# Attention on one core: the first group's inverse from 16x16 blocks, and paced first loads

## The chip, the core and the metric

One Trainium2 chip, and of it one core. Its engines run side by side, each through its own queue in order: TensorE (matrix products, PE in the profile, its weight loads PEld), VectorE (DVE), ScalarE (ACT), GpSimd (POOL) and SyncE (SP), which here issues the DMA transfers. They wait for each other by semaphores. The measure is the device time of one execution in microseconds; three runs stand at 898.11, 903.13 and 903.36, so the median is 903.13.

## The reference, cut to what matters

Attention with a delta rule runs ahead of two feed-forward stages, which the change doesn't touch. Batch 4, 8 heads, 768 tokens, head size 48:

```
k_n = k / (norm(k) + 1e-06)
for t in range(S):
    y[t] = q[t] @ state
    v_old = k_n[t] @ state
    state = state + beta[t] * outer(k_n[t], v[t] - v_old)
```

Its output, the heads side by side, goes into a spectral mixer with a feed-forward part (`mixer`) and then into a gated feed-forward part (`gated`).

## The kernel before, in words

`attention` works in chunks of C = 64 tokens. A chunk of one head is solved in closed form: with G the products of its normalised keys (a gram matrix), the recurrence inside it is a unit lower triangular system, whose inverse T is needed before anything of the chunk can be computed. Two heads stand on the 128 partitions, U = 32 units (pairs of head and chunk) make a group, and there are six groups. A 64x64 inverse is made of four quarters of 32 rows: two diagonal 32x32 blocks, and a corner that comes from them by two products on TensorE.

Ahead of the main loop, and for later groups within it:

- `piece("g", g, p)` (line 423) multiplies a quarter of a group's keys with themselves, the gram; `piece("a", g, p)` keys with queries, the score. Each is 16 matmuls of 64x64, into one of two PSUM banks that take turns by the list `uses`. ScalarE drains each (lines 314 and 318).
- `to_lanes` (558) transposes the diagonal blocks, gathered in `g_diag`, so that each of 32 units times 4 quarters has a lane of its own. Group 0's blocks are copied out of `gram_sb` by VectorE (618), ScalarE (353) and GpSimd (282), later groups' by DMA (`diagonal`, 185).
- `lanes` finds the norms (ScalarE gives the root, 307) and scales; `column` (599, 603) then solves the 32x32 blocks by forward substitution, 31 columns of two operations each, every one waiting for the one before it through the semaphore `chain`. In column 24 (`AHEAD`), `to_lanes` of the next group is done. `unlanes` (610, 612) transposes back into `t_rows` and `t_cols`.
- `couple_w` (435) and `couple_x` (448) form the corner on TensorE, in halves of 16 units; ScalarE puts the parts into `tt` (325, 336, 346).

The main loop has 48 steps, 8 for each group, on TensorE and ScalarE: u (492), y (509, 514), s (527) and r (474) of four units a step, each drained by ScalarE. VectorE meanwhile does the inverse of group g + 1. Blocks and couplings of later groups stand between the steps: at group 0's steps only `g` blocks of group 3 and, at the last step, `couple_w(1, 0)`. SyncE's list of loads is written by hand, each held back by a `wait_ge` on what frees its buffer or on a place in `chain`. GpSimd masks the scores (`causal`, 246), scales v (`scaled`, 253) and clears `t_lane` (`clear`, 260).

## Time and profile before

| | |
|---|---|
| median of three runs | 903.13 us (898.11 to 903.36) |
| profiled execution, its own time | 899.3 us |
| its span | 897.5 us |
| mean granted TensorE clock | 0.928 |
| attention, first to last step | up to about 260 us |
| group 0's inverse on VectorE | 13.2 to 49.1 us |
| group 0's steps on TensorE | 58.4 to 79.7 us |

The span is that of the instructions; the execution's own time has what lies around it as well. In the profile an instruction has a start and a duration in microseconds, and the engine's idle time ahead of it with what ended it. A granted clock of 1.00 is TensorE's 2.4 GHz, 0.50 its 1.2 GHz. A 32-bit matmul shows as two records, so 16 matmuls are 32 records.

### The profile page before, as it was taken

The numbers are of one execution on the slowest core, as the hardware profiler recorded it, in microseconds if no ns is written. First come the engines' busy times: TensorE is split into PE (matmuls) and PEld (weight loads), VectorE is DVE, ScalarE is ACT, GpSimd is POOL, SyncE is SP. The second block draws the span as 40 slices with busy tenths as digits, with TensorE's granted clock in tenths as the row PEclk, the third lists the DMA queues.
The fourth block names the chain that finished last, engine by engine and source line by source line (L and its number), as shares of the span: only waits on it lengthen the run. The fifth ranks groups of instructions, "written<-read, shape, count | busy, mean of one in ns | idle before, by whom it ended". The sixth has DMA issues, their size and how long they took to land.

```text
span 897.5 us, 24703 instructions
## 1 busy us (share of the span) xinstructions
PE 834.6 (93%) x10634; PEld 809.9 (90%) x10634; DVE 475.1 (53%) x1092; ACT 301.3 (34%) x654; POOL 199.4 (22%) x167
## 2 busy tenths in 40 slices
PE   7368999999984999999999999999999999999998
PEld 6368989899884999999999999999899899899898
DVE  5999999999295554435443443333632432432421
ACT  4246575675431221122111211123441431431421
POOL 3123123023001803600540000000132222222231
PEclk9758779697886999999999999999999999999999
DMA  6633454422564030012000103003410010000001
GB/s 198 163 121 99 148 148 119 132 58 74 158 215 131 3 123 19 18 54 70 18 18 14 56 18 116 20 15 105 152 53 27 27 53 27 26 0 27 27 1 53
DMA packets 38074, 65.14 MB, mean 73 GB/s; under 512 B 4249, under 2 KB 26082, under 8 KB 37986
## 3 DMA queue, kind: packets, MB, share of 16 engines
q1 hardware_dynamic: 37986, 63.85, 22.7%
q8 instruction: 69, 1.13, 0.5%
q14 instruction: 19, 0.16, 0.1%
HBM read 46.86 MB, written 14.16 MB: 68 GB/s over the span
## 4 chain that ended last, share of the span: by engine, by line
PE 61%; issue 20%; DVE 11%; ACT 4%; POOL 2%; DMA 1%; SPq 1%; POOLq 0%; ACTq 0%; DVEq 0%
PE m_ps_h L1111 13%; PE g_ps_v L1622 11%; PE m_ps_d L1111 11%; PE ps_ga L423 4%; PE g_ps_y L1622 3%; PE g_ps_u L1622 3%; PE ps_y L509 3%; PE ps_y L514 2%; PE ps_u L492 2%; DVE t_lane L603 2%; DVE prod L599 2%; PE ps_r L474 2%; ACT tt L346 2%; PE ps_s L527 2%; POOL g_vn_lo L1519 2%
## 5 line engine op out<-in xcount | busy, mean ns | idle before, releaser
L1111 PE MATMUL m_ps_h<-m_unt_hi,m_w_hi 128*128 128x256 f32 x432 | 122.7, 284 | 2.1 <-DVE m_unt_lo L1301 2.1
L1111 PE MATMUL m_ps_h<-m_unt_lo,m_w_hi 128*128 128x256 f32 x432 | 121.9, 282 | 0.0
L1111 PE MATMUL m_ps_h<-m_unt_hi,m_w_lo 128*128 128x256 f32 x432 | 121.8, 282 | 0.0
L1307 DVE SCALAR_TENSOR_TENSOR m_h_lo<-m_ps_h,m_h_hi 128x512 fp32r<-128x512 f32 x72 | 49.8, 692 | 107.8 <-ACT m_h_hi L1011 107.8
L1111 PE MATMUL m_ps_d<-m_w_hi,m_h_hi 128*128 128x384 f32 x288 | 97.6, 339 | 0.0
L1111 PE MATMUL m_ps_d<-m_w_hi,m_h_lo 128*128 128x384 f32 x288 | 96.4, 335 | 0.0
L1111 PE MATMUL m_ps_d<-m_w_lo,m_h_hi 128*128 128x384 f32 x288 | 96.3, 334 | 0.0
L1011 ACT ACTIVATE m_h_hi<-m_ps_h 128x512 fp32r<-128x512 f32 x72 | 43.1, 598 | 151.0 <-PE m_ps_h L1111 151.0
L1111 PEld LDWEIGHTS m_ps_h<-m_unt_hi,m_w_hi 128*128 128x128 f32 x432 | 82.4, 191 | 2.6 <-DVE m_unt_lo L1301 2.5
L1111 PEld LDWEIGHTS m_ps_h<-m_unt_hi,m_w_lo 128*128 128x128 f32 x432 | 83.5, 193 | 0.0
L1111 PEld LDWEIGHTS m_ps_h<-m_unt_lo,m_w_hi 128*128 128x128 f32 x432 | 82.5, 191 | 0.0
L603 DVE TENSOR_TENSOR t_lane<-t_lane,prod 128x31 f32<-128x31 f32 (+15 forms) x186 | 66.3, 356 | 6.4
L423 PE MATMUL ps_ga<-kq 64*64 64x64 f32 x1536 | 59.4, 235 | 10.6 <-DMA kq<-kq_g 8.3
L599 DVE TENSOR_TENSOR prod<-g_lane,t_lane 128x31 f32<-128x31 f32 (+15 forms) x186 | 63.7, 343 | 6.2
L1783 DVE TENSOR_TENSOR g_vs<-g_ps_v,g_bias 128x384 f32<-128x384 f32 x32 | 17.9, 558 | 92.3 <-PE g_ps_v L1622 92.0
L1519 POOL TENSOR_TENSOR g_vn_lo<-g_vn,g_vn_hi 128x512 fp32r<-128x512 f32 x24 | 30.5, 1286 | 161.5 <-ACT g_vn_hi L1561 161.5
L423 PEld LDWEIGHTS ps_ga<-kq 64*64 64x64 f32 x1536 | 56.2, 150 | 11.2 <-DMA kq<-kq_g 4.4
L1622 PE MATMUL g_ps_v<-g_ws_hi,g_vn_hi 128*128 128x384 f32 x192 | 64.4, 335 | 0.0
L1622 PE MATMUL g_ps_v<-g_ws_hi,g_vn_lo 128*128 128x384 f32 x192 | 64.1, 334 | 0.0
L1622 PE MATMUL g_ps_v<-g_ws_lo,g_vn_hi 128*128 128x384 f32 x192 | 64.1, 334 | 0.0
L1525 POOL TENSOR_TENSOR g_g<-g_vs,g_ut 128x384 f32<-128x384 f32 x32 | 36.7, 1147 | 114.0 <-DVE g_vs L1783 114.0
L514 PE MATMUL ps_y<-u_sb,score 64*64 64x48 f32 x768 | 60.9, 246 | 0.0
(220 smaller groups left out, 1963.5 us busy)
## 6 DMA issues: line engine op xcount, KB each, us to landing
kq<-kq_g SPq DMA_DIRECT2D x48, 256.0 KB, 3.6
v_in<-v_g SPq DMA_DIRECT2D x12, 384.0 KB, 4.2
k_in<-k_g SPq DMA_DIRECT2D x12, 384.0 KB, 3.6
x_scr<-y_sb SPq DMA_DIRECT2D x24, 192.0 KB, 2.9
stage<-w_ch SPq DMA_DIRECT2D x6, 768.0 KB, 4.8
x_scr<-m_x_sb SPq DMA_DIRECT2D x24, 192.0 KB, 1.9
g_x<-x_scr SPq DMA_DIRECT2D x24, 192.0 KB, 4.5
out<-g_y SPq DMA_DIRECT2D x24, 192.0 KB, 1.9
```

The lines of the kernel that those rows point to most:

```text
L346: last = act.activation(tt[g % 2][quarter(a), :, H * (a % 2):H * (a % 2) + H], t_cols[quarter(a)], ACT.Copy)
L423: last = pe.matmul(ps_ga[m % 2][lo:lo + C, C * j:C * j + C], x[:, 0], x[:, 0 if what == "g" else 1], start=True, stop=True)
L509: pe.matmul(ps_y[out, at:at + D], kq[g % 4][lo:lo + C, 1, PR * m + j], s_sb[lo:lo + C, b, j], start=True, stop=False)
L514: last = pe.matmul(ps_y[out, at:at + D], score[g % 2][rows, PR * m + j], u_sb[rows, j0 % 2, j], start=j0 < NB, stop=True)
L599: dve.tensor_tensor(x, g_lane[g % 2][:, j + 1:H, j].unsqueeze(2).broadcast_to([P, m, n]), t_lane[:, j, 0:n].unsqueeze(1).broadcast_to([P, ...
L603: dve.tensor_tensor(below, below, x, ALU.add).then_inc(chain, 1)
L1011: act.activation(h_hi[:, 2 * g:2 * g + 2], ps_h[g % 2][:, :].rearrange("p (f t) -> p f t", f=2), ACT.Relu).then_inc(h_hi_ok, 1)
L1111: last = pe.matmul(out, first[x], second[y], start=(k == 0 and m == 0), stop=(k == n - 1 and m == 2))
L1307: dve.scalar_tensor_tensor(h_lo[:, 2 * g:2 * g + 2].rearrange("p f t -> p (f t)"), ps_h[g % 2][:, :], 0.0, h_hi[:, 2 * g:2 * g + 2].rearra ...
L1519: pool.tensor_tensor(vn_lo[:, t], vn[:, t % 2], vn_hi[:, t].bitcast(F32), ALU.subtract).then_inc(vn_lo_ok, 1)
L1525: pool.tensor_tensor(g[:, n % 2], vs[:, n % 2], ut[:, f, HS * h:HS * h + HS], ALU.mult).then_inc(g_ok, 1)
L1622: last = pe.matmul(out, first[x], second[w], start=(k == 0 and m == 0), stop=(k == n - 1 and m == 2))
```

## The change

Group 0 alone gets another inverse. Its four gram blocks have a PSUM bank each (`ps_four`, four banks that `ps_y` and the two turning banks lie in), and VectorE and ScalarE copy the diagonal blocks straight out of them, half by half, before ScalarE drains the grams. VectorE's lanes invert only the two 16x16 blocks on the diagonal of each 32x32 block (`fine_column`, 15 columns instead of 31, both blocks in one operation). With D their inverse and L the block below them, TensorE forms V = I - L D (`fine_v`) and then D V (`fine_inverse`), which is the 32x32 inverse, and its transpose for two quarters. ScalarE's `below` makes L out of `g_diag` by a factor of -1 or 0 for each partition.

Only the first half of group 0's units gets all that ahead of the loop. The second half's `fine_v`, `fine_inverse`, `couple_w` and `couple_x` stand at steps 1 to 4 of it. So do the four score blocks of group 1, at steps 2 to 5. The first loads go in pairs, each pair waiting for the landing of the pair two before it; the loads of group 1's queries come after them. `to_lanes(1)` follows `unlanes(0)`. The table that the square root needs is loaded at the start. The rest of the kernel is as it was.

```diff
-    FIRST = (("g", 0), ("a", 0), ("g", 1), ("a", 1), ("g", 2))
+    FIRST = (("g", 0), ("g", 1), ("a", 0), ("g", 2))
...
+        def links(g):
+            return FINE_LINKS + (g - 1) * LINKS if g else 0
...
+            sp.wait_ge(kq_in[0][0][0], 32)
+            for s, g in ((0, 1), (1, 0), (0, 2)):
+                for c in range(2):
+                    sp.wait_ge(kq_in[0 if (s, g) == (0, 1) else 1 if s else 0][0 if s or g == 1 else 1][c], 32)
+                    for p in (2 * c, 2 * c + 1):
+                        load_kq(g, s, p)
+            sp.wait_ge(kq_in[2][0][1], 32)
             diagonal(1)
...
+            for p in range(4):
+                sp.wait_ge(chain, links(1) + 2 + 6 * p)
+                load_kq(1, 1, p)
...
-                pool.wait_ge(chain, g * LINKS + 2 * AHEAD + 4)
+                pool.wait_ge(chain, links(g) + 2 * AHEAD + 4 if g else links(1))
...
+            act.wait_ge(one_ok, 1)
+            act.activation(one[:, 1:2], one[:, 0:1], ACT.Sqrt)
+            for c in range(2):
+                act.wait_ge(ga_done, 2 * c + 2)
+                for a in (1, 3):
+                    act.activation(g_diag[quarter(a), HU * c:HU * c + HU], first_gram(quarter(a), c, 1),
+                                   ACT.Copy).then_inc(dg_act, 1)
+            act.wait_ge(dg_dve, 4)
             for p in range(4):
                 piece("g", 0, p)
-            act.wait_ge(ga_out, 4)
-            act.activation(g_diag[quarter(1)], gram_sb[0][quarter(1), 1], ACT.Copy).then_inc(dg_act, 1)
+            roots(0)
...
+            def fine_v(c):
+                m = turn["v", 0, c]
+                bank_free(m)
+                pe.matmul(ps_ga[m % 2][:, 0:HU * H], ident[:], unit[:].unsqueeze(1).broadcast_to([P, HU, H]),
+                          start=True, stop=False, skip_group_check=True)
+                pe.wait_ge(below_ok, 1)
+                pe.wait_ge(trows_ok, 1)
+                for j in range(HU):
+                    for a in range(4):
+                        u = HU * c + j
+                        last = pe.matmul(coupling(m, quarter(a))[:, j], below[quarter(a), u], t_rows[quarter(a), u],
+                                         start=False, stop=True, skip_group_check=True)
+                last.then_inc(ga_done, 1)
+            def fine_inverse(c):
+                m = turn["c", 0, c]
+                bank_free(m)
+                pe.wait_ge(tcols_ok, 1)
+                pe.wait_ge(ga_out, turn["v", 0, c] + 1)
+                for j in range(HU):
+                    for a in range(4):
+                        u = HU * c + j
+                        last = pe.matmul(coupling(m, quarter(a))[:, j], v_fine[quarter(a), u], t_cols[quarter(a), u],
+                                         start=True, stop=True)
+                last.then_inc(ga_done, 1)
+                m = turn["r", 0, c]
+                bank_free(m)
+                for j in range(HU):
+                    for a in (0, 2):
+                        u = HU * c + j
+                        last = pe.matmul(coupling(m, quarter(a))[:, j], t_cols[quarter(a), u], v_fine[quarter(a), u],
+                                         start=True, stop=True)
+                last.then_inc(ga_done, 1)
...
+                if k == 1:
+                    fine_v(1)
+                if k == 2:
+                    fine_inverse(1)
+                if 2 <= n < 6 and i + 1 < G:
                     piece("a", i + 1, n - 2)
...
-                if i and n == 1:
+                if n == (1 if i else 3):
                     couple_w(i, 1)
-                if i and n == 2:
+                if n == (2 if i else 4):
                     couple_x(i, 1)
...
+            def fine_column(j):
+                m, n = Q - 1 - j, j + 1
+                x = prod[:, 0:2 * m * n].rearrange("p (b i k) -> p b i k", b=2, k=n)
+                g, t = diagonal_pair(g_lane[0]), diagonal_pair(t_lane)
+                rest = t[:, :, j + 1:Q, 0:n]
+                dve.tensor_tensor(x, g[:, :, j + 1:Q, j].unsqueeze(3).broadcast_to([P, 2, m, n]),
+                                  t[:, :, j, 0:n].unsqueeze(2).broadcast_to([P, 2, m, n]), ALU.mult).then_inc(chain, 1)
+                dve.wait_ge(chain, 2 * j + 3)
+                dve.tensor_tensor(rest, rest, x, ALU.add).then_inc(chain, 1)
+                dve.wait_ge(chain, 2 * j + 4)
```

TensorE from its first instruction to the loop's first three steps, before the change (`ps_ga<-kq` are the blocks, `ps_u`, `ps_y`, `ps_s` the steps):

```order
L423 MATMUL ps_ga<-kq 64x64 x320
L435 MATMUL ps_ga<-t_rows,gram_sb 32x32 x64
L448 MATMUL ps_ga<-t_cols,w_sb 32x32 x64
L492 MATMUL ps_u<-v_in,tt 64x48 x16
L514 MATMUL ps_y<-u_sb,score 64x48 x8
L527 MATMUL ps_s<-u_sb,k_in 48x48 x8
L492 MATMUL ps_u<-v_in,tt 64x48 x8
```

and with the change, as far as the second u (`w_sb` under line 546 is `below`, `score` under 559 and 567 is V):

```order
L500 MATMUL ps_four<-kq 64x64 x256
L539 MATMUL ps_four<-unit,ident 128x512
L546 MATMUL ps_four<-t_rows,w_sb 32x32 x64
L559 MATMUL ps_four<-t_cols,score 32x32 x64
L567 MATMUL ps_four<-score,t_cols 32x32 x32
L515 MATMUL ps_four<-t_rows,gram_sb 32x32 x32
L531 MATMUL ps_four<-t_cols,w_sb 32x32 x32
L612 MATMUL ps_u<-v_in,tt 64x48 x8
L539 MATMUL ps_four<-unit,ident 128x512
L546 MATMUL ps_four<-t_rows,w_sb 32x32 x64
L612 MATMUL ps_u<-v_in,tt 64x48 x8
```

Sixty-four of the score blocks' matmuls have left the start, half of the couplings too, and the first `fine` products stand ahead of the loop, the others between its first two u.

TensorE, steps 2 to 4 of group 0 before the change, from the second y:

```order
L514 MATMUL ps_y<-u_sb,score 64x48 x8
L527 MATMUL ps_s<-u_sb,k_in 48x48 x8
L466 MATMUL ps_r<-v_in,ident 128x192
L474 MATMUL ps_r<-s_sb,kq 64x48 x8
L492 MATMUL ps_u<-v_in,tt 64x48 x8
```

and with the change, from the first y:

```order
L634 MATMUL ps_four<-u_sb,score 64x48 x8
L647 MATMUL ps_s<-u_sb,k_in 48x48 x8
L559 MATMUL ps_four<-t_cols,score 32x32 x64
L567 MATMUL ps_four<-score,t_cols 32x32 x32
L500 MATMUL ps_four<-kq 64x64 x16
L612 MATMUL ps_u<-v_in,tt 64x48 x8
L634 MATMUL ps_four<-u_sb,score 64x48 x8
L647 MATMUL ps_s<-u_sb,k_in 48x48 x8
L500 MATMUL ps_four<-kq 64x64 x16
L515 MATMUL ps_four<-t_rows,gram_sb 32x32 x32
L586 MATMUL ps_r<-v_in,ident 128x192
L594 MATMUL ps_r<-s_sb,kq 64x48 x8
```

Between the steps stand now the other half of `fine_inverse`, two score blocks of group 1 and the coupling.

ScalarE at steps 3 and 4 of group 0 with the change (`u_sb`, `s_sb`, `y_sb`, `r_sb` are a step's drains, line 405 is `first_corners`, line 371 `solved_x`):

```order
L360 ACTIVATE w_sb<-ps_four 128x512 [waits ga_done]
L405 ACTIVATE tt<-t_cols 32x16x32 [waits tt_zero,ga_out]
L405 ACTIVATE tt<-t_cols 32x16x32 x3
L437 ACTIVATE r_sb<-ps_r 128x192 [waits p_done]
L441 ACTIVATE u_sb<-ps_u 128x192 [waits u_done]
L337 ACTIVATE ps_r<-v_in 128x192 [waits r_ok]
L453 ACTIVATE s_sb<-ps_s 128x192 [waits s_done]
L458 ACTIVATE y_sb<-ps_four 64x2x4x48 [waits y_done]
L353 ACTIVATE score<-ps_four 128x512 [waits ga_done]
L349 ACTIVATE gram_sb<-ps_four 128x8x2x32 [waits ga_done]
L371 ACTIVATE tt<-ps_four 32x16x32 [waits tt_zero,ga_done]
```

The four corner copies stand ahead of step 4's drains; before the change they, and every coupling drain of group 0, stood ahead of the loop.

## Rows read from the trace of the kernel before

**Rows 1.** The page's part 1: busy us, share of the span, instructions.
```profile
PE 834.6 (93%) x10634; PEld 809.9 (90%) x10634; DVE 475.1 (53%) x1092; ACT 301.3 (34%) x654; POOL 199.4 (22%) x167
```

**Rows 2.** Busy time by stretches: length; PE, PEld, DVE, ACT, POOL; clock, DMA share, GB/s.
```profile
45.20:58.30 13.10, 6.90 (x256) 6.79 (x256) 12.25 (x29) 7.64 (x10) 5.92 (x5) 0.50 0.19 62
58.30:70.10 11.80, 11.33 (x199) 10.56 (x201) 10.91 (x27) 4.08 (x12) 0.00 (x0) 0.50 0.57 175
70.10:79.60 9.50, 9.50 (x337) 9.42 (x333) 8.78 (x23) 6.56 (x19) 3.01 (x2) 1.00 0.45 134
...
81.20:101.50 20.30, 19.33 (x507) 18.76 (x509) 18.79 (x49) 12.06 (x24) 4.08 (x4) 0.58 0.46 136
...
120.00:160.30 40.30, 37.22 (x1155) 36.02 (x1154) 37.33 (x93) 25.37 (x59) 8.75 (x6) 0.83 0.44 128
```

**Rows 3.** Waits of TensorE, us in total, times, longest: 0 to 250, then 83.3 to 230.
```profile
PE ps_ga L435 <- DVE t_rows L610: 15.2, 2, 13.3
...
PE ps_u L492 <- ACT tt L346: 4.4, 4, 2.0
```

**Rows 4.** TensorE in order of time: start, duration, line, what, and its wait.
```profile
16.13 3.95 PE L423 MATMUL ps_ga<-kq 64*64 64x64 f32 x128 [0.74 <-ACT score L318]
...
28.64 5.50 PE L423 MATMUL ps_ga<-kq 64*64 64x64 f32 x128 [3.88 <-DMA kq<-kq_g]
47.42 3.47 PE L435 MATMUL ps_ga<-t_rows,gram_sb 32*32 32x32 f32 x122 [13.29 <-DVE t_rows L610]
...
58.35 1.09 PE L492 MATMUL ps_u<-v_in,tt 64*64 64x48 f32 x16 [4.03 <-ACT tt L346]
...
79.09 0.57 PE L423 MATMUL ps_ga<-kq 64*64 64x64 f32 x11
81.52 1.20 PE L435 MATMUL ps_ga<-t_rows,gram_sb 32*32 32x32 f32 x64 [1.86 <-DVE t_rows L610]
```

**Rows 5.** GpSimd and ScalarE in order of time, at group 2's inverse.
```profile
117.53 0.95 POOL L260 MEMSET t_lane<- 128x1024 f32 x1 [0.29 <-DVE t_cols L612]
...
122.02 2.11 ACT L346 ACTIVATE tt<-t_cols 32x1024 f32<-32x1024 f32 x2
```

**Rows 6.** VectorE in order of time, group 0's inverse.
```profile
10.99 2.13 DVE L618 COPY g_diag<-gram_sb 32x1024 f32<-32x1024 f32 x2 [8.98 <-ACT gram_sb L314]
...
15.63 0.35 DVE L568 RECIPROCAL rinv<-root 128x32 f32<-128x32 f32 x1 [0.30 <-ACT root L307]
...
17.72 1.22 DVE L589 SCALAR_TENSOR_TENSOR g_lane<-g_lane,scale 128x1024 f32<-128x1024 f32 x1
...
19.46 0.22 DVE L599 TENSOR_TENSOR prod<-g_lane,t_lane 128x60 f32<-128x60 f32 x1
19.71 0.22 DVE L603 TENSOR_TENSOR t_lane<-t_lane,prod 128x60 f32<-128x60 f32 x1
...
21.16 0.30 DVE L599 TENSOR_TENSOR prod<-g_lane,t_lane 128x135 f32<-128x135 f32 x1
21.50 0.30 DVE L603 TENSOR_TENSOR t_lane<-t_lane,prod 128x135 f32<-128x135 f32 x1
...
45.23 2.05 DVE L610 STREAM_TRANSPOSE t_rows<-t_lane 128x1024 f32<-128x1024 f32 x1
```

**Rows 7.** ScalarE in order of time: block drains, then corner drains.
```profile
30.19 0.60 ACT L314 ACTIVATE gram_sb<-ps_ga 128x512 f32<-128x512 f32 x1 [4.80 <-PE ps_ga L423]
31.90 0.60 ACT L314 ACTIVATE gram_sb<-ps_ga 128x512 f32<-128x512 f32 x1 [1.11 <-PE ps_ga L423]
...
53.71 2.40 ACT L336 ACTIVATE tt<-ps_ga 32x512 f32<-32x512 f32 x4
```

**Rows 8.** The page's part 6: DMA issues, KB each, us to landing.
```profile
kq<-kq_g SPq DMA_DIRECT2D x48, 256.0 KB, 3.6
```

**Rows 9.** GpSimd in order of time: the scaling of v for group 0.
```profile
38.98 2.77 POOL L253 TENSOR_TENSOR v_in<-v_in,norm 128x1536 f32<-128x1536 f32 x1 [26.40 <-DVE t_lane L603]
```

205 lines of the change are left out of this document (135 added, 70 removed).

## The prediction

> **What bounds the kernel now.** The page comes first. TensorE is busy 93% of the span and VectorE 53% [rows 1]. The edit touches only the first 120 us or so, and those shares say nothing of that stretch, so the next view is the table by stretches. In 58.3 to 70.1 and 70.1 to 79.6 TensorE is busy nearly throughout, first at a granted clock of 0.50 (1.2 GHz), then at 1.00 (2.4 GHz), while VectorE is busy over 90% as well [rows 2]. Busy shares can't tell which of the two sets the end. The list of waits can: TensorE waited for VectorE's `t_rows` twice, 13.3 us and 1.9 us (15.2 less 13.3), and from 83.3 to 230 us never again; there it waits for ScalarE's corner copies, 4.4 us over 4 waits [rows 3]. The 13.3 us end at 47.42, where group 0's inverse is ready, and the 1.86 us at 81.52, for group 1's [rows 4]. At group 2, VectorE's `t_cols` were done at 117.5 (GpSimd's clear of `t_lane` starts on them), and ScalarE came to its copies at 122.02 [rows 5]: VectorE is 4.5 us early. So VectorE bounds the program up to 81.5 us, and TensorE from there. **A VectorE that is 16 us earlier is worth only what TensorE can follow.** The quantity to forecast is when TensorE reaches the first matmul of `couple_w(1, 0)`, now 81.52. Everything behind it moves by the same amount.
>
> **VectorE, group 0.** It now waits for the last gram drain, then copies two 32x1024 quarters in 2.13 us, 10.99 to 13.12 [rows 6]; with 0.6 us for that drain the fourth block is done near 10.4. After: the first half is copied while the other is still being multiplied, and only two 32x512 copies from PSUM follow 10.4. ScalarE takes 2.40 us for four of that size [rows 7], 0.6 each, so 11.6, which is 1.5 us earlier. The square root then stands behind ScalarE's four gram drains (four in 2.2 us, 0.6 each less some overlap), so `rinv` starts at 14.1 where 15.63 stood: still 1.5. The two 16x16 scalings have 256 elements a lane each where 1024 took 1.22 us; a quarter of the elements twice saves 0.3 to 0.4. The columns: 62 operations with `to_lanes(1)` between them ran from 18.94 to 45.23. The new chain has 30 operations of 30 to 128 elements. Operations of 60 and 135 elements take 0.22 and 0.30 us, 0.25 and 0.34 from start to start [rows 6]; thirty at 0.245 to 0.325 make 8.6 us. So columns run 17.1 to 25.7, `t_rows` is ready at 27.8 (now 47.3), `t_cols` at 29.7. `to_lanes(1)`, 2.9 us, now follows instead of lying inside. Group 1's columns thus start some 16 us earlier. The 4-dimensional patterns of `fine_column` are in no row; were each operation 0.1 us slower, the chain would be 3 us longer, which then ties with the next item.
>
> **Loads.** In pairs that wait for each other, each about 3.6 us from issue to landing [rows 8], two pairs are under way at a time: landings near 4.4, 5, 8, 9, 11.5, 12.5, 15, 16. The uses (first blocks at 4.4, the second group's at 14, the last at 24) come later, so I take the pacing at nothing. What it could give is an earlier first block (a few tenths), what it could cost a late `diagonal(1)`, which sends four transfers and is queued behind the last pair and the drain of group 1's grams at about 20. Its data is needed at 29.7, so 7 us of cover. The v loads land near 27 and `scaled(0)` (2.77 us [rows 9]) lies beside the transposes; its `v_ok` is needed at 43. `load_kq(1, 1)` moved behind `chain` 34 (near 37), done landing by 45, needed at 48.
>
> **TensorE before the loop.** After the four gram blocks it stands until ScalarE has drained them (13.8). Then twelve blocks at 0.99 us (3.95 for four) plus 1.5 us for a start at 1.2 GHz, as after the gap before 28.64 [rows 4], then the 128x512 identity matmul, 1.35 us scaled from 192 columns: 28.6. So VectorE's result at 27.8 is no longer what it waits for. Now the join for half the units. Price: `couple_w(1, 0)`, 32 matmuls shown as 64 records, took 1.20 us at 2.4 GHz; 128 records took 3.47 at 1.2 GHz [rows 4], so 18.8 or 27 ns a record. `fine_v` (128 records) 2.4, copy 0.7, `fine_inverse` (192) 3.6 to 5.2, three copies 1.8 (0.6 each [rows 7]), `couple_w` 1.4, copy 0.6, four corner copies 2.4 covering `couple_x`, two more 1.2: 14.3 to 16, starting at 28.6. First u matmul at 43.5, where it was 58.35. Bounds: 41 if four corners at once run faster than two, 46 all at 1.2 GHz.
>
> **TensorE's loop over group 0.** It now takes 58.35 to 79.66, 528 records of 64-row matmuls. Moved in: four `a` blocks of group 1, 128 records; `fine_v(1)` and `fine_inverse(1)`, 320; `couple_w(0, 1)` and `couple_x(0, 1)`, 128; the second identity matmul. That is 656 of the one kind and 448 of the other. Rates: 337 records in 9.5 us at 2.4 GHz [rows 2], 35.5 a us; at 1.2 GHz one block of 32 per 1.71 us (the drains at 30.19 and 31.90 [rows 7]), 18.8 a us. At 2.4 GHz throughout: 18.5 + 8.4 + 1.4 + 0.5 (the 192-column identity matmul) = 28.8 us. At 1.2 GHz: 34.9 + 12.1 + 2.7 + 1.0 = 50.7 us. The trace has the loop at 1.2 GHz until 70.1, about 10 us behind its dense start at 60, and the next stretch, 81.2 to 101.5, averages 0.58, so 17 of its 20 us [rows 2]. I take 10 us: they do a fifth of the work, the rest takes 23.1, together 33.1. New waits, from ScalarE's order: the `a` block behind `fine_inverse(1)` waits for the `t_cols` copy (0.7); `couple_x(0, 1)` and the fifth u matmul wait behind the four corner copies that ScalarE does first, 1.3 and 0.6; 0.4 more for the rest. 3 us. So 43.5 + 33.1 + 3 = 79.6 against 81.5: **1.9 us gained.** Behind the next boundary, from 120 to 160.3, the clock averages 0.83: 13.7 us at 1.2 GHz, against 17 behind this one, which has the 1.86 us gap that now goes. I take 1 us for it (0 to 2). VectorE's group 1 is done at about 68 (its `unlanes` waits for `couple_x(0, 1)`, near 64), group 2 starts when ScalarE gives the root at step 6, near 70 where it was 83: 12 us early, not binding. The total is 3 us.
>
> The profiled run took 899.3, so 896.3 by its own sum. It lies 3.8 under the median of 903.13, and one of the three runs at 898.11; 903.1 - 3 = **900**.
>
> The Trainium skill ("TensorEngine Tiling (Array Packing)", Key Properties) says that 32x32 tiles execute independently and that a change of tiling mode drains TensorE. No row has four corners at once. By the first, 256 of the 320 fine records would shrink; by the second, the eight new switches between 64 and 32 rows in the loop would each cost something, against this change.
>
> **Rivals.**
> (1) Four corners overlap: if 256 records in each half take half as long, 2.4 us go from the start and 2.4 to 3.5 from the loop, and with the higher clock from 4 us on (as at 28.64) the loop takes 30.5: 40.9 + 30.5 - 3 + 3 = 71.4, a gain of 10 to 11 with the 1: 892. For it: four disjoint corners of the array. Against: two already alternate, and 18.8 ns may be the floor. 0.15. The page named above would have this.
> (2) Only the clock is better: high after 4 us, 43.5 + 30.5 + 3 = 77, gain 5.5: 897.5. 0.2.
> (3) VectorE's 16 us come through whole: 887. It would need TensorE's added work to be free; [rows 2] has no idle time for it. 0.04.
> (4) **Slower, by the clock in the loop.** The 32-row matmuls from 47.42 on ran at 0.50 to their end, 7 us of them [rows 2, 4]. In the loop they now stand at its beginning. If 1.2 GHz lasts t us, the loop ends at 43.5 + 3 + 28.8 + 0.43 t, which passes 81.5 at t = 14.4. With t = 25 it is 86, 4.6 later: 908 (0.17). With the whole loop at 1.2 GHz, 97.2, so 919 (0.05).
> (5) The early change doesn't do what it says: a paced load comes late at start, and VectorE's chain with it; up to 3 us at the start leaves about 0: 903. 0.04.
> The forecast has 0.35.
>
> **Numbers.** 1% is 9 us, about what a measurement can tell from no change. Faster by more: (3), most of (1), a little of (2), 0.21. Slower by more: (4)'s second case and a tail of its first, 0.08. Between: 0.71. The range takes in (1) with a little beyond and the first case of (4): 890 to 908.
>
> **What would show it.** The first u matmul near 43.5; `t_rows` at 28; `couple_w(1, 0)` near 79.6 with no wait for `t_rows` ahead of it; group 0's loop some 36 us long, of which 10 at 1.2 GHz; VectorE waiting for ScalarE's root, and idle more than before. Wrong if TensorE still waits for `t_rows` of group 1, if a fine record takes other than 18.8 to 27 ns, or if the stretch behind group 1 changes length by over 2 us.

## The result and the profile after

The changed kernel took 906.87 us (median of 20 runs, 900.66 to 910.82); the kernel before, on the same chip, 902.0 (20 runs, 897.22 to 907.13). The ratio is 1.0052, with a 95% interval of 1.003 to 1.0073: about 4.7 us slower, where 3 us of gain were forecast. The time lies inside the range, on the other side of no change. The profiled execution has a span of 905.3 against 897.5.

VectorE first, since the change is made for it: in order of time, start, duration, line, operation, then its wait.

```profile
12.10 1.93 DVE L681 STREAM_TRANSPOSE g_lane<-g_diag 128x1024 f32<-128x1024 f32 x1
...
16.65 0.75 DVE L717 SCALAR_TENSOR_TENSOR g_lane<-g_lane,scale 128x256 f32<-128x256 f32 x2
17.43 0.21 DVE L739 TENSOR_TENSOR prod<-g_lane,t_lane 128x30 f32<-128x30 f32 x1
...
21.80 0.29 DVE L742 TENSOR_TENSOR t_lane<-t_lane,prod 128x128 f32<-128x128 f32 x1
...
26.12 2.08 DVE L749 STREAM_TRANSPOSE t_rows<-t_lane 128x1024 f32<-128x1024 f32 x1
28.10 1.91 DVE L751 STREAM_TRANSPOSE t_cols<-t_lane 128x1024 f32<-128x1024 f32 x1
...
64.27 0.19 DVE L730 TENSOR_TENSOR t_lane<-t_lane,prod 128x31 f32<-128x31 f32 x1
74.78 2.05 DVE L749 STREAM_TRANSPOSE t_rows<-t_lane 128x1024 f32<-128x1024 f32 x1 [10.33 <-PE ps_four L531]
...
83.25 0.35 DVE L691 RECIPROCAL rinv<-root 128x32 f32<-128x32 f32 x1 [4.59 <-ACT root L342]
```

Beside [rows 6], `t_rows` of group 0 is ready at 28.2 in place of 47.3. The four-dimensional patterns of `fine_column` cost nothing extra (30 elements in 0.21 us, 128 in 0.29). VectorE ends group 1's columns at 64.46. It then waits 10.33 us for TensorE's `couple_x(0, 1)` and 4.59 us for ScalarE's root, and group 2 starts at 83.25, where it started before the change too. The whole lead is gone there, in waits for TensorE and for ScalarE behind it.

TensorE in order of time. The rows answer to [rows 4]; x is the number of records, and each f32 matmul shows as two.

```profile
28.47 0.95 PE L546 MATMUL ps_four<-t_rows,w_sb 32*32 32x32 f32 x89
31.40 0.54 PE L546 MATMUL ps_four<-t_rows,w_sb 32*32 32x32 f32 x39 [1.97 <-issue]
32.72 1.25 PE L559 MATMUL ps_four<-t_cols,score 32*32 32x32 f32 x89 [0.79 <-ACT score L388]
36.29 0.74 PE L559 MATMUL ps_four<-t_cols,score 32*32 32x32 f32 x37 [2.31 <-issue]
...
36.84 1.90 PE L567 MATMUL ps_four<-score,t_cols 32*32 32x32 f32 x63
40.59 1.92 PE L515 MATMUL ps_four<-t_rows,gram_sb 32*32 32x32 f32 x64 [1.84 <-ACT t_rows L396]
43.28 1.92 PE L531 MATMUL ps_four<-t_cols,w_sb 32*32 32x32 f32 x64 [0.78 <-ACT w_sb L360]
46.87 1.09 PE L612 MATMUL ps_u<-v_in,tt 64*64 64x48 f32 x16 [1.68 <-issue]
...
53.94 0.90 PE L559 MATMUL ps_four<-t_cols,score 32*32 32x32 f32 x83
57.70 0.80 PE L559 MATMUL ps_four<-t_cols,score 32*32 32x32 f32 x43 [2.86 <-issue]
...
76.01 0.57 PE L612 MATMUL ps_u<-r_sb,tt 64*64 64x48 f32 x13 [0.74 <-issue]
...
86.36 1.07 PE L515 MATMUL ps_four<-t_rows,gram_sb 32*32 32x32 f32 x56
```

The join starts when it was forecast to, at 28.47. Three times it stops in the middle of a run of equal matmuls, 1.97, 2.31 and 2.86 us long, with no releaser ("issue"). From 31.40 to 36.29 lie 39 + 89 = 128 records. (The 1.68 us ahead of the first u matmul are named "issue" as well, but are the wait for ScalarE's last two corner copies. So are the 0.74 us ahead of the fifth u matmul at 76.01: ScalarE's copies of the second half end at 75.92.)

```profile
74.73 1.19 ACT L371 ACTIVATE tt<-ps_four 32x512 f32<-32x512 f32 x2 [0.82 <-PE ps_four L531]
```

`couple_w(1, 0)`, whose first matmul the forecast was about, starts at 86.36. It stood at 81.52 in [rows 4], and 79.6 was forecast. Busy time by stretches, the join and then the loop over group 0: length; PE, PEld, DVE, ACT, POOL (instructions); clock, DMA share, GB/s.

```profile
28.40:46.80 18.40, 9.10 (x449) 8.37 (x448) 16.61 (x38) 6.53 (x12) 8.19 (x6) 0.62 0.28 87
46.80:86.40 39.60, 33.63 (x1110) 30.87 (x1112) 23.14 (x52) 19.26 (x46) 8.74 (x6) 0.79 0.40 122
```

The same loop before the change, with less in it:

```profile
58.30:81.50 23.20, 20.89 (x530) 19.99 (x531) 21.59 (x50) 11.24 (x32) 4.91 (x3) 0.74 0.50 153
```

TensorE is idle 9.3 us of the join's 18.4 and 6.0 us of the loop's 39.6. The page's part 3 (DMA queue, its kind: packets, MB, share) has 69 packets of instructions before:

```profile
q8 instruction: 69, 1.13, 0.5%
```

and 74 after:

```profile
q8 instruction: 74, 1.21, 0.6%
```

Part 1 has 11278 TensorE records in place of the 10634 in [rows 1]: 644 more, and five packets more. That is one packet of 16 KB for each 129 records, or 128 within what so small a count can tell. The theory taken into the experiments is **A**: TensorE's instructions come in such pieces, and a piece that is worked off faster than the next one comes leaves TensorE standing.

### The profile page after: what moved, and what is told of

Its sections match the earlier page's. It is cut to its first block, busy times and chain, and to the rows that moved or that the text cites. A ratio compares the mean times of both kernels' runs of the same rounds, so it can differ in the third digit from the quotient of the medians.

```text
span 905.3 us, 25993 instructions
## 1 busy us (share of the span) xinstructions
PE 840.6 (93%) x11278; PEld 812.0 (90%) x11278; DVE 463.0 (51%) x1069; ACT 307.3 (34%) x670; POOL 200.3 (22%) x171
## 4 chain that ended last, share of the span: by engine, by line
PE 65%; issue 22%; ACT 5%; DVE 4%; POOL 2%; DMA 1%; SPq 1%; POOLq 0%; ACTq 0%; DVEq 0%
PE m_ps_h L1262 12%; PE g_ps_v L1773 11%; PE m_ps_d L1262 10%; PE ps_four L500 5%; PE g_ps_y L1773 3%; PE ps_u L612 3%; PE ps_four L634 3%; PE ps_four L629 3%; PE ps_r L594 2%; PE ps_four L515 2%; POOL g_vn_lo L1670 2%; PE ps_s L647 2%; PE g_ps_u L1773 2%; ACT tt L381 2%; PE ps_four L531 1%
## 5 line engine op out<-in xcount | busy, mean ns | idle before, releaser
L1162 ACT ACTIVATE m_h_hi<-m_ps_h 128x512 fp32r<-128x512 f32 x72 | 43.1, 598 | 150.9 <-PE m_ps_h L1262 150.9
L1262 PEld LDWEIGHTS m_ps_h<-m_unt_hi,m_w_lo 128*128 128x128 f32 x432 | 83.3, 193 | 0.0
L500 PE MATMUL ps_four<-kq 64*64 64x64 f32 x1536 | 57.2, 228 | 10.5 <-DMA kq<-kq_g 4.7
L500 PEld LDWEIGHTS ps_four<-kq 64*64 64x64 f32 x1536 | 53.8, 144 | 11.1 <-DMA kq<-kq_g 4.7
L634 PE MATMUL ps_four<-u_sb,score 64*64 64x48 f32 x768 | 60.8, 243 | 2.1 <-issue 2.0
L730 DVE TENSOR_TENSOR t_lane<-t_lane,prod 128x31 f32<-128x31 f32 (+15 forms) x155 | 56.6, 365 | 5.3
L727 DVE TENSOR_TENSOR prod<-g_lane,t_lane 128x31 f32<-128x31 f32 (+15 forms) x155 | 56.6, 365 | 5.2
```

The costliest lines, as they stand in the source:

```text
L500: last = pe.matmul(ps[lo:lo + C, C * j:C * j + C], x[:, 0], x[:, 0 if what == "g" else 1], start=True, stop=True)
L634: last = pe.matmul(ps_y[out, at:at + D], score[g % 2][rows, PR * m + j], u_sb[rows, j0 % 2, j], start=j0 < NB, stop=True)
L727: dve.tensor_tensor(x, square(g_lane[g % 2])[:, j + 1:H, j].unsqueeze(2).broadcast_to([P, m, n]), t[:, j, 0:n].unsqueeze(1).broadcast_to([ ...
L730: dve.tensor_tensor(rest, rest, x, ALU.add).then_inc(chain, 1)
L1162: act.activation(h_hi[:, 2 * g:2 * g + 2], ps_h[g % 2][:, :].rearrange("p (f t) -> p f t", f=2), ACT.Relu).then_inc(h_hi_ok, 1)
L1262: last = pe.matmul(out, first[x], second[y], start=(k == 0 and m == 0), stop=(k == n - 1 and m == 2))
```

## The experiments

Group 0 in each profile, in us. "Stops" are the pauses named "issue" between `t_rows(0)` and the first u matmul, without the one directly ahead of it. Each ratio is to the kernel before as it ran beside that row, on the same chip (medians of 902.0 to 903.9); medians of different rows are compared by their ratios.

| kernel | stops in the join | first u | `couple_w(1, 0)` | median | ratio to before (95%) |
|---|---|---|---|---|---|
| before | 0 | 58.35 | 81.52 | 902.0 | |
| after | 4.28 | 46.87 | 86.36 | 906.87 | 1.0052 (1.0030 to 1.0073) |
| a_shift1 | 4.16 | 49.26 | 88.95 | 909.32 | 1.0074 (1.0044 to 1.0103) |
| b_shift1 | 0 | 58.32 | 81.49 | 906.37 | 1.0031 (1.0014 to 1.0048) |
| b_shift2 | 0 | 58.00 | 81.17 | 906.75 | 1.0031 (1.0014 to 1.0047) |
| b_early | 0 | 57.23 | 80.35 | 902.84 | 0.9981 (0.9961 to 1.0001) |
| a_piece | 4.67 | 47.68 | 85.61 | 907.6 | 1.0043 (1.0019 to 1.0066) |
| a_late_g2 | 1.55 | 43.78 | 91.31 | 911.92 | 1.0111 (1.0067 to 1.0155) |
| a_whole | 8.74 | 56.45 | 82.74 | 906.05 | 1.0042 (1.0013 to 1.0072) |
| a_cut | 4.36 | 47.81 | 81.51 | 901.66 | 0.9994 (0.9969 to 1.0019) |
| a_calm | 3.85 | 47.19 | 85.31 | 905.82 | 1.0042 (1.0016 to 1.0069) |
| a_late_calm | 1.84 | 44.73 | 87.93 | 910.16 | 1.0079 (1.0058 to 1.0100) |
| a_serial | 1.16 | 53.32 | 100.12 | 921.13 | 1.0202 (1.0178 to 1.0227) |
| a_nopace | 1.23 | 42.76 | 80.82 | 909.74 | 1.0090 (1.0060 to 1.0119) |
| a_bf16 | 0.49 | 41.87 | 75.81 | 898.27 | 0.9959 (0.9933 to 0.9985) |
| a_busy | 5.06 | 48.88 | 83.72 | 908.19 | 1.0062 (1.0034 to 1.0090) |
| a_nopace_calm | 3.73 | 45.52 | 82.69 | 904.1 | 1.0020 (1.0000 to 1.0040) |
| b_early_calm | 0 | 58.46 | 81.55 | 900.68 | 0.9988 (0.9967 to 1.0008) |
| a_bf16_rows | 1.24 | 42.62 | 77.83 | 900.75 | 0.9979 (0.9960 to 0.9998) |
| a_bf16_best | 1.01 | 40.36 | 75.84 | 899.43 | 0.9963 (0.9943 to 0.9983) |

The time follows `couple_w(1, 0)` through most of the table: set against the changed kernel, 13.8 us later in a_serial is 13.5 us by the ratios, 10.5 earlier in a_bf16 is 8.4. a_nopace, whose profile is not one of its usual executions, is the exception. The positions are of one execution each, and executions of one kernel differ by 5 to 10 us, so single rows can be off by a few us. From `couple_w(1, 0)` to `couple_w(5, 0)` the two kernels' profiles take 149.0 and 152.4 us. But b_early, which leaves TensorE's work as it was, takes 152.7, and the kernels of the table lie between 149.0 and 154.2 there: the 3 us that the first pair seems to lose are within the spread of executions.

### Where the pieces end: a_shift1, b_shift1, b_shift2, b_early

One block of `("g", 2)` is multiplied twice (b_shift2 two of them), which only moves the ends of the pieces.

```
-                for j in range(QU):
+                again = 2 if (what, g, p) == ("g", 2, 3) else 1
+                for j in [j for _ in range(again) for j in range(QU)]:
```

> The changed kernel, with the 16 matmuls of the last block ahead of the join (group 2's fourth gram block) done twice, 32 matmul records more, the same result. Theory A (supply): TensorE's program reaches it in pieces of 128 matmul records, and a piece that is worked off faster than the next one comes leaves TensorE standing at the piece's end. Then the stop inside the first fine_v, now after 89 of its 128 records, comes after 57, the one inside fine_inverse moves up by 32 too, and the later pauses move with them; the time may change by up to 3 us either way. Theory B (the products themselves, four corners into one PSUM bank): the stops stay where they are, after 89 records, and the time stays 0.5% above the kernel before, plus at most 0.9 us.

> The kernel before, with the same 16 matmuls twice: 0.9 us (1.7 at the lower clock) in a stretch where TensorE then waits 13 us for VectorE, so their own cost is nothing. Theory A: the pauses in the loops of groups 1 to 5 that nothing in the profile explains (5.7 us from 120 us on in the kernel before) fall elsewhere; their sum may become anything from 3 to 12 us, and the time follows it. Theory B: 1.000 of the kernel before, within 0.2%.

> The kernel before, with those 16 matmuls three times, 64 records more. Theory A: as with 32 records more, at other places: another sum of pauses, so a time that differs from both by 1 to 4 us. Theory B: 1.000, within 0.2%.

TensorE in order of time, in a_shift1:

```profile
30.63 0.69 PE L547 MATMUL ps_four<-t_rows,w_sb 32*32 32x32 f32 x57
33.27 0.81 PE L547 MATMUL ps_four<-t_rows,w_sb 32*32 32x32 f32 x71 [1.96 <-issue]
34.87 0.97 PE L560 MATMUL ps_four<-t_cols,score 32*32 32x32 f32 x57 [0.79 <-ACT score L388]
36.97 1.17 PE L560 MATMUL ps_four<-t_cols,score 32*32 32x32 f32 x69 [1.13 <-issue]
```

The stops stand behind 57 records of `fine_v` and of `fine_inverse` where they stood behind 89: 32 records more ahead of the join, and each stop comes 32 records sooner in it. A stop belongs to a place in the stream of instructions, not to a matmul. The sixteen matmuls are some 1 us of work, and the first u comes 2.4 us later; 2.2 of these lie ahead of the join, which starts at 30.63. Before the change, where TensorE waits 13 us anyway, they move neither the first u nor `couple_w(1, 0)`. Yet b_shift1 and b_shift2 are both 0.31% slower than before, with no difference to be seen up to group 1. What lies behind that is not settled. The pauses named "issue" from 80 to 262 sum to 9.8 and 12.7 us there, against 5.7 in the profile of before. That could come from the places of the piece ends, but b_early has 10.5 with the places of before, and is not slower.

b_early is the kernel before with the first group's direct copies from PSUM and the early table load alone (a part of the edit):

```
+                for a in (0, 2):
+                    dve.tensor_copy(g_diag[quarter(a), HU * c:HU * c + HU],
+                                    first_gram(quarter(a), c, 0)).then_inc(dg_dve, 1)
```

> The kernel before with one part of the change alone: group 0's diagonal blocks copied out of four PSUM banks before the gram drains, and the table of the square root loaded at the start. The 32x32 inverse, the loads and the loop stay. VectorE's chain starts 1.1 us earlier in the changed kernel (12.10 for 13.16), and in the kernel before it bounds the program up to 81.5 us, with TensorE 1.86 us ahead of it. So 1.1 us faster, 0.9988, if nothing else moves. By theory A the order of TensorE's instructions is hardly shifted and no pause is added. If the early part is what costs, it would be slower than the kernel before, 1.002 or more.

It brings `couple_w(1, 0)` forward by 1.17 us and the time by 0.19%, at the edge of what can be measured (the interval takes in no change). So the early part of the change costs nothing, and the loss lies in what the other parts add.

### A piece in an idle gap, and a piece out of the way: a_piece, a_late_g2

a_piece adds 64 idle matmuls where TensorE waits for ScalarE:

```
+                if what == "g" and g == 0:
+                    for j in range(U):
+                        for lo in HEADS:
+                            x = kq[0][lo:lo + C, 0, j]
+                            pe.matmul(ps_u[lo:lo + C, 0:C], x, x, start=True, stop=True)
```

> 64 more matmuls (64x64, written to a bank that nobody reads; 128 records of the trace, since each f32 matmul shows as two) right behind the first group's four blocks, where TensorE waits 3.60 us for ScalarE (14.21). At 30 ns a record they fit that wait. Theory A (TensorE's instructions come to it in pieces of 128 records, one in about 4 us, and the early stretch is bound by that): the blocks end 3 to 4 us later, the stops of 1.97 and 2.31 us in the join stay, the first u matmul comes at 50 to 51 in place of 46.87 and couple_w(1,0) at 89.5 to 90.5 in place of 86.36; time 909 to 911. Theory B (the stops belong to the 32x32 matmuls themselves, the supply is no bound): first u at 47.2, couple_w(1,0) at 86.7, time as before this edit, 907.

Theory A as it stood falls here: `couple_w(1, 0)` is not later, and the first u by 0.8 us only, so the numbers are those of theory B. B itself, that the stops belong to the 32-row matmuls, had fallen with a_shift1. At 32 ns a record (the 128 added ones ran in 4.12 us) a piece comes in time. Between 10 and 28 us the supply adds no more than the stops of 0.82 and 0.49 us, which the changed kernel has there too (0.89 and 0.49). It binds where records go faster than that.

a_late_g2 takes group 2's four gram blocks from ahead of the join into the loop (a part of the edit):

```
-    FIRST = (("g", 0), ("g", 1), ("a", 0), ("g", 2))
+    FIRST = (("g", 0), ("g", 1), ("a", 0))
+    LATE = {0: (0,), 1: (1, 2), 3: (3,)}
```

> The four blocks of group 2's gram (128 records, one piece) go from ahead of the join into the step loop: p0 at step 0, p1 and p2 at step 1, p3 at step 3. Theory A: TensorE waits from about 25 to 28.2 for t_rows while the pieces ahead are already there, so the join loses the stops of 1.97 and 2.31 us: first u at 42.5 to 43.5 in place of 46.87; the loop takes one piece more, so couple_w(1,0) at 83 to 84.5; time 903 to 905. Theory B: the stops stay, first u at 46.9, the loop is 3 to 4 us longer, couple_w(1,0) at 89.5, time 910.

TensorE in order of time, in a_late_g2:

```profile
28.06 1.34 PE L552 MATMUL ps_four<-t_rows,w_sb 32*32 32x32 f32 x128 [3.69 <-DVE t_rows L758]
30.18 1.46 PE L565 MATMUL ps_four<-t_cols,score 32*32 32x32 f32 x90 [0.78 <-ACT score L391]
33.18 0.70 PE L565 MATMUL ps_four<-t_cols,score 32*32 32x32 f32 x35 [1.55 <-issue]
...
43.78 1.07 PE L618 MATMUL ps_u<-v_in,tt 64*64 64x48 f32 x16
...
56.58 0.72 PE L653 MATMUL ps_s<-u_sb,k_in 64*48 64x48 f32 x12 [5.76 <-issue]
```

The same `fine_v` matmuls, started after a wait of 3.69 us, run through without a stop: 128 records in 1.34 us. So the stop doesn't belong to them. The first u comes 3.1 us earlier, as A said. But then a stop of 5.76 us stands in the loop, in the middle of 64-row matmuls of the old kind, and the kernel is slower than the changed one. The DMA queues of a_late_g2 in 44 to 54 (slices in tenths, then the queues):

```profile
DMA  9400009397899988994659848999999999976531
...
q1 hardware_dynamic: 1218, 2.46, 79.2%
```

No row for instructions: for ten microseconds no piece arrived, while data took 79% of the DMA engines' time. That gave **theory D**: a piece waits behind data transfers.

### More or less work at the join: a_whole, a_cut

a_whole puts both halves of the join ahead of the loop (PE's part shown; ScalarE's order follows it):

```
             fine_v(0)
+            fine_v(1)
             fine_inverse(0)
+            fine_inverse(1)
             couple_w(0, 0)
+            couple_w(0, 1)
             couple_x(0, 0)
+            couple_x(0, 1)
```

> The second half's fine_v, fine_inverse, couple_w and couple_x go from steps 1 to 4 of the loop to ahead of it, beside the first half's. 900 records stand then between 28.47 and the first u. Theory A: seven pieces of 3.7 to 4.3 us, first u at 55 to 58, then 23.2 us as the loop took before the change plus 2 to 3 for the four score blocks that it still holds: couple_w(1,0) at 81 to 83.5, time 902 to 904. Theory B (busy times and waits on ScalarE alone: 16.5 us of matmuls at the rows' durations and some 2 us of waits): first u at 47 to 49, couple_w(1,0) at 73 to 77, time 893 to 898.

The first u at 56.45, as A had it (55 to 58), against 47 to 49 from the matmuls' own time; five stops sum to 8.74 us. The loop then takes 26.3 us. `couple_w(1, 0)` at 82.74 is in A's bounds, the time of 906.05 is 2 us over them.

a_cut leaves out 256 records of the second half's fine work. A part of group 0's inverse is then missing, so it only shows what that work costs:

```
-                for j in range(HU):
+                for j in range(0 if c else HU):
```

(in `fine_v`, and likewise to one matmul in the columns' part of `fine_inverse`).

> The second half's 64 fine_v matmuls, 63 of its 64 matmuls for the columns and one of its 32 for the rows are left out (part of the computation is missing): 256 records, exactly two pieces, so that all later piece ends fall where they did. Theory A, the loop of group 0 is bound by the supply: couple_w(1,0) 6.5 to 8.5 us earlier, at 78 to 80, time 898 to 900. Rival C, the loop is bound by the chain of waits between TensorE and ScalarE from step to step, and the fine work lies partly beside it: 3 us or less, couple_w(1,0) at 83.4 or later, time 904 or more.

It is 4.85 us earlier at `couple_w(1, 0)` and 5.2 us in time: between A's 6.5 and the 3 of the rival, and enough to be level with before. Counted from the first u, the loop is 5.8 us shorter, where the changed kernel has 3.6 us of these matmuls and the stop of 2.86: they have next to no cover in the loop.

### Corner by corner: a_serial

```
-                for j in range(HU):
-                    for a in range(4):
+                for a in range(4):
+                    for j in range(HU):
```

> The changed kernel, with fine_v and fine_inverse written corner by corner (all 16 units of one 32-row quarter, then the next), so that neighbouring matmuls do not lie on different quarters. Theory A (instruction pieces set the pace of the join): 128 records take 3 to 4 us in place of 1.5, but the stops of 1.97, 2.31 and 2.86 us shrink by as much; first u at 46.5 to 48.5, couple_w(1,0) at 86 to 88, time 906 to 909. Rival (the overlap of the four corners is what keeps the join short): every group of 128 costs 2 us more, six of them and the rows' part, stops unchanged: first u at 50.5 to 51.5, couple_w(1,0) at 92 to 94, time 912 to 914.

The orders of the loops are swapped in `fine_v` and in both parts of `fine_inverse`. It is a clear miss for A, and 6 to 7 us beyond the rival's numbers too. The stops shrink from 4.28 to 1.16 us, but the matmuls take far longer (TensorE in a_serial):

```profile
28.96 2.80 PE L546 MATMUL ps_four<-t_rows,w_sb 32*32 32x32 f32 x89
32.92 2.00 PE L546 MATMUL ps_four<-t_rows,w_sb 32*32 32x32 f32 x39 [1.16 <-issue]
35.70 6.28 PE L559 MATMUL ps_four<-t_cols,score 32*32 32x32 f32 x125 [0.78 <-ACT score L388]
```

89 records took 0.95 us with neighbours on different corners and 2.80 us on the same one: the four corners do overlap, 10.7 ns a record against 31.5. So the supply isn't all: the stops shrink by 3.1 us and the join is 6 us longer. A slower matmul is paid for by a shorter stop only as long as it keeps up with the pieces.

### Transfers beside the pieces: a_calm, a_late_calm, a_busy

a_calm moves the `kq(2, 1)` loads (1 MB) from steps 0 and 1 to steps 4 to 7; a_late_calm does so in a_late_g2; a_busy moves them, and the v(1) loads, ahead to 29 us, beside the join.

```
-                if n < 2 and g + 2 < G:
-                    for p in ((2 + n,) if g else (2 * n, 2 * n + 1)):
-                        load_kq(g + 2, 1, p)
+                if g and n < 2 and g + 2 < G:
+                    load_kq(g + 2, 1, 2 + n)
+                if g == 0 and n >= 4:
+                    load_kq(2, 1, n - 4)
```

> The changed kernel, but the four loads of kq(2,1) (256 KB each) go from steps 0 and 1 of the loop to steps 4 to 7; TensorE's work is not touched. Theory D (an instruction piece of TensorE waits behind the data transfers of the stretch 46 to 56, where the DMA share is 0.85 to 1.04): the stop of 2.86 us at 57.70 shrinks below 1.3, couple_w(1,0) comes 1.5 to 2.5 us earlier than 86.36, time 904 to 905.5. If the transfers have nothing to do with it: stop 2 to 3 us, couple_w(1,0) at 86 to 86.7, time 907.

> The kernel with group 2's gram blocks in steps 0, 1 and 3 of the loop, and with the kq(2,1) loads at steps 4 to 7 (and the diagonal of group 2 behind the loads of step 3). Theory D: the stop of 5.76 us at 56.58, ahead of which no instruction packet was seen from 43 to 54 while the DMA share was 0.94 to 1.00, falls to 2 or less; first u at 43.8 as without the load edit; couple_w(1,0) at 91.31 less 4 to 6 and less the 2.18 us wait for a late load: 83 to 86, time 902 to 906. If the transfers have nothing to do with it: stop 5 to 6, couple_w(1,0) at 89 to 91, time 909 to 912.

> The changed kernel with the loads of v(1) (2 of 384 KB) and kq(2,1) (4 of 256 KB) moved from steps 0 and 1 of the loop to right behind v(0), at about 29, where the DMA is quiet from 30 to 38 and the join runs. Theory D (an instruction piece waits behind data transfers): the stops of 1.97 and 2.31 us in the join grow to 3 or more in all over what they were (sum 6 to 8), first u at 48.5 to 50.5, while the stop at 57.70 shrinks to 2 or less; time 906 to 909. If the transfers have nothing to do with it: first u at 46.5 to 47.5, all stops as they were, 907.

TensorE in a_late_calm, at the place of the 5.76 us:

```profile
53.62 0.47 PE L656 MATMUL ps_s<-u_sb,k_in 64*48 64x48 f32 x12 [1.53 <-issue]
```

The DMA queues of a_late_calm in 44 to 54:

```profile
q1 hardware_dynamic: 769, 1.66, 52.2%
q8 instruction: 2, 0.03, 1.2%
```

1.66 MB of data in place of 2.46, two instruction packets in place of none, and the stop falls from 5.76 to 1.53 us: that is what D expected of the stop (2 or less). `couple_w(1, 0)`, 3.4 us earlier at 87.93, and the time of 910.16 are better than without the edit, but miss the 83 to 86 and 902 to 906 that were expected. In a_calm the stop at 57.70 becomes one of 2.01 us at 56.58, not one below 1.3, and `couple_w(1, 0)` gains 1.05 us, not 1.5 or more. Nor does the 2.01 tell anything by itself: in a_piece, with the loads where the changed kernel has them, the same stop is 1.84.

```profile
57.38 0.78 PE L559 MATMUL ps_four<-t_cols,score 32*32 32x32 f32 x43 [1.84 <-issue]
```

TensorE in a_busy, the join's second stop and the place of the changed kernel's third:

```profile
38.30 0.74 PE L562 MATMUL ps_four<-t_cols,score 32*32 32x32 f32 x37 [3.13 <-issue]
...
56.64 0.56 PE L562 MATMUL ps_four<-t_cols,score 32*32 32x32 f32 x43 [0.17 <-issue]
```

With the data beside the join its stop grows from 2.31 to 3.13, and the later one, now in a quiet stretch, falls from 2.86 to 0.17 (another of 0.84 us comes at 60.55). Both signs are D's. The first stands against 1.89 to 2.52 in the changed kernel, a_calm, a_cut and a_piece, whose join is the same, the second against 1.84 to 2.86. The sizes are smaller than expected (the join's stops sum to 5.06, not 6 to 8), and the times say little: a_calm is 0.1% below the changed kernel, a_busy 0.1% above, both within the intervals.

The traces settle more than these sizes do. They hold the time at which each instruction packet moves, here found in windows of 0.1 us:

| kernel | packet at | stop ends at | us between | length of the stop |
|---|---|---|---|---|
| after | 29.1 | 31.40 | 2.3 | 1.97 |
| after | 33.6 | 36.29 | 2.7 | 2.31 |
| after | 55.5 | 57.70 | 2.2 | 2.86 |
| a_busy | 35.9 | 38.30 | 2.4 | 3.13 |
| a_busy | 54.4 | 56.64 | 2.2 | 0.17 |
| a_late_g2 | 54.3 | 56.58 | 2.3 | 5.76 |
| a_late_calm | 51.3 | 53.62 | 2.3 | 1.53 |
| a_whole | 35.1 | 37.78 | 2.7 | 2.62 |
| a_bf16 | 29.9 | 32.26 | 2.4 | 0.49 |

Stops from 0.17 to 5.76 us long all end 2.2 to 2.9 us behind a packet; so do the others looked up in a_calm, a_shift1, a_nopace, a_piece, a_cut and a_serial. What ends a stop is thus the packet ahead of it, and this holds for theories A and D alike: a piece that comes late. In a_late_g2 the packet ahead of that at 54.3 moved at 43.1. TensorE had stood since 50.82, while data held the DMA engines. Where these are quiet, packets follow each other in 3.4 to 3.9 us at the closest (54.4 and 57.8 in a_busy, 33.6 and 37.3 in the changed kernel). But the 2.2 to 2.9 us between packet and matmul are no waiting for data. In the join's second stop nothing moves at all (share and GB/s are the last two):

```profile
33.97:36.29 2.32, 0.01 (x2) 0.00 (x2) 2.22 (x5) 0.00 (x0) 2.32 (x3) 0.50 0.00 0
```

### The paced first loads: a_nopace, a_nopace_calm

```
-            sp.wait_ge(kq_in[0][0][0], 32)
```

(and the wait inside the loop over the six pairs of loads that follow).

> The changed kernel without SP's six waits for landings among the first loads; the loads' order stays. Theory A: the paced loads cost nothing on the path of the join: first gram block at 4.4 to 4.8 as in both kernels, t_rows(0) within 1 us of 28.2, couple_w(1,0) within 1 us of 86.36, time 905.5 to 908. Rival (the pacing holds loads back and is part of the loss): TensorE's blocks end 1 to 3 us earlier and couple_w(1,0) comes 1.5 to 3 us earlier, time 903 to 905. Or the pacing protects the first blocks: first gram block 1 to 3 us later, time 908 to 910.

Its profiled execution, at 901.32 us, is the fastest of its five, which go up to 914.28. In that one the case that was forecast comes true (TensorE in a_nopace):

```profile
28.09 1.28 PE L544 MATMUL ps_four<-t_rows,w_sb 32*32 32x32 f32 x128 [1.40 <-DVE t_rows L747]
30.16 0.94 PE L557 MATMUL ps_four<-t_cols,score 32*32 32x32 f32 x89 [0.79 <-ACT score L386]
32.34 0.55 PE L557 MATMUL ps_four<-t_cols,score 32*32 32x32 f32 x37 [1.23 <-issue]
```

The blocks end at 25.6, without the two stops of 0.89 and 0.49 us that the changed kernel has in them. TensorE waits for `t_rows`, one stop of the join is gone, the first u comes at 42.76 and `couple_w(1, 0)` at 80.82. Why the other four executions took 907 to 914 no profile here shows. So neither the expectation of no difference nor one of the two others holds for both the profile and the median; the median, 909.74, gives no sign that the waits cost time.

> The changed kernel without SP's waits among the first loads, and with the loads of kq(2,1) at steps 4 to 7. The one without waits alone had 901.32 us in its profiled execution (first u 42.76, couple_w(1,0) 80.82) and 907 to 914 in the four others. Theory D says that the others had pieces held up by the loads of steps 0 and 1: then this one has a median of 901 to 905 and few executions over 907. If the spread comes from the first loads themselves: median 907 to 910, again with a spread of over 8 us.

The median is 904.1 (12 runs, 898.17 to 906.6), and none of its executions goes over 907, as D expects. That lies 0.3% below the changed kernel by the ratios, whose intervals touch.

### Half the records, the same matmuls: a_bf16, a_bf16_rows, a_bf16_best

In a_bf16, `fine_v` and the columns' part of `fine_inverse` read the upper half of each f32 word as bf16, so that each matmul shows as one record:

```
+        def high(x):
+            return x.bitcast(BF16)[:, 1::2]
```

> The changed kernel; the 32x32 matmuls of fine_v and of fine_inverse's columns read the upper half of each f32 word as bf16, so that each shows as one record in place of two (the operands are cut to bf16, the products are coarser; all matmuls still stand there). 4 times 64 records less, two pieces exactly. Theory A2 (a piece of 128 records takes TensorE 4 to 5 us at least, so records and not matmuls are what the join and the loop of group 0 pay): the stops of 1.97 and 2.31 us mostly go, first u at 43.5 to 44.5 in place of 46.87, couple_w(1,0) 4.5 to 6.5 us earlier, at 80 to 82, time 900 to 902.5. Rival (only the matmuls' own time is saved, 0.6 to 1 us for each of the four): first u at 45 to 45.5, couple_w(1,0) at 83 to 84, time 903.5 to 905.

TensorE in order of time, in a_bf16:

```profile
29.96 0.66 PE L550 MATMUL ps_four<-t_rows,w_sb 32*32 32x32 bf16 x64
31.45 0.32 PE L563 MATMUL ps_four<-t_cols,score 32*32 32x32 bf16 x25 [0.83 <-ACT score L392]
32.26 0.45 PE L563 MATMUL ps_four<-t_cols,score 32*32 32x32 bf16 x39 [0.49 <-issue]
...
41.87 1.09 PE L616 MATMUL ps_u<-v_in,tt 64*64 64x48 f32 x16 [1.68 <-issue]
...
48.03 0.73 PE L563 MATMUL ps_four<-t_cols,score 32*32 32x32 bf16 x64
```

Here 64 matmuls take 0.66 to 0.77 us, where the same ones took 1.5 to 2 us. Over the four runs of 64 that saves some 4 us of the matmuls' own time. But `couple_w(1, 0)` comes 10.55 us earlier, though the join starts 1.5 us later. From the first fine matmul to `couple_w(1, 0)` it is 12.0 us less: 5.2 of TensorE's busy time and 6.8 of idle time. Most of the latter is stops: 4.28 to 0.49 us in the join, and the 2.86 us in the loop are gone (one of 1.05 us comes later). It is more than A2 expected (4.5 to 6.5 us), and three times the rival's 2.4 to 3.4, which would have been some 4 with the matmuls' own time as it came out. At 0.9959 of before it has the lowest ratio of the table; its products are coarser.

> As the kernel whose fine_v and column matmuls read bf16 halves, and the rows' matmuls (32 in each half) too: 128 records less again, so 384 in all, three pieces. Theory A2 (records are what is paid, and 256 of them gave 10.5 us at couple_w(1,0) and 8.4 us in time): first u 1.5 to 2.5 us before 41.87, couple_w(1,0) 3 to 5 us before 75.81, at 71 to 73, time 894 to 896. Rival (the loop of group 0 is by now bound by its chain from step to step, and group 1 by VectorE's columns, done at 64.46 after the change): couple_w(1,0) at 74 to 75.5, time 897 to 898.5.

> The same, without SP's waits among the first loads and with the kq(2,1) loads at steps 4 to 7, which took 2 to 3 us off the changed kernel together. If the two gains add: 891.5 to 894, first u at 38 to 39. If few stops are left for them to take away: within 1 us of the kernel without them, 894 to 897.

In a_bf16_rows, 128 records fewer gave nothing more (77.83 and 900.75, against 75.81 and 898.27). A2's 71 to 73 is missed by 5 us, and the rival's 74 to 75.5 by 2. The median moves the same way, by ratios of 0.9979 and 0.9959. So the number of records alone doesn't set the price. The idle time from 42.62 to 77.83 is 5.3 us, where a_bf16 has 2.8, so the reading that the gain ends once the stops are short is possible, but this pair of profiles doesn't show it; that of a_bf16_rows is its slowest execution, 903.77. a_bf16_best, 899.43, is level with both; the gains don't add.

### The early part with later loads: b_early_calm

> The kernel before, with the direct copies of the first group's diagonal blocks from PSUM and the early table load alone (0.9981 of before), and with the loads of kq(2,1) at steps 4 to 7 of group 0. Theory D: the loop of group 0 has no stop here to take away, so at most the later loads shift: 0.996 to 1.000 of before, 899 to 903. If kq(2,1) comes late for its score blocks in group 1: slower, 903 to 906.

The ratio is 0.9988 (0.9967 to 1.0008): no different from before, nor from b_early.

## Why the prediction was wrong, point by point

**VectorE, group 0: right.** `t_rows` ready at 28.2 (forecast 27.8), `t_cols` at 30.0 (29.7). Group 1's first column is at 38.24 in place of 53.06, 15 us earlier (16).

**What bounds: right.** TensorE no longer waits for `t_rows(1)` at `couple_w(1, 0)`; VectorE waits, idle 15 us more. Its lead is worth only what TensorE can follow. When VectorE would start on group 2 was wrong, though without a price: near 70 was forecast, and it was 83.25, since `couple_x(0, 1)` came at 73.48 and not near 64.

**TensorE before the join: right by luck.** It started at 28.47, where 28.6 was forecast. The forecast had 1.5 us for a start at 1.2 GHz; the granted clock was 1.00 all through 14.2 to 28.4, and two stops among the blocks, 0.89 and 0.49 us, stood in that place.

**TensorE from the join to the first u: the step that failed.** It took 18.4 us where 14.9 were forecast, from 28.6 to 43.5. (The steps that the prediction lists add up to 14.1 to 15.7, where it says 14.3 to 16.) The waits for ScalarE are 5.1 (0.79, 1.84, 0.78, 1.68), where the steps had 4.3; the matmuls 9.1 where they had 10.6 (the four corner copies that cover `couple_x` counted as matmuls), since the corners overlap. The missing term is the stops, 4.28 us. The prediction priced a record by its duration alone, 18.8 to 27 ns. Fine records run in 10.7 ns and are then paid for at their piece's end. From one stop's end to the next are 4.9 us for 128 records, 38 ns each, with a wait of 0.79 us for ScalarE among them. Rival 1 was thus half right: the corners overlap, and the time is not gained. By the prediction's own sign, a record outside 18.8 to 27 ns, it was wrong here.

**The loop: the same term.** It was forecast at 36.1 us and measured at 39.5. Busy time is 33.6 against the forecast 33.1, by luck: two errors cancel. The clock averages 0.79, so some 16.6 us at 1.2 GHz in place of 10 (0.21 of 39.6 us over a half). And the fine records took 15 ns at that clock, not 27. At the prediction's 0.43 us for each us at the low clock, the first cost 2.8 us, and the second gave back about as much. Idle time is 6.0 us where 3 were given. It is 2.4 us of waits for ScalarE (0.69 for the `t_cols` copy, 1.01 ahead of `couple_x(0, 1)`, 0.74 ahead of the fifth u), of which the forecast had 0.7, 1.3 and 0.6, and 3.5 us of stops (2.86, 0.60). Nothing is left over for the eight changes between 64 and 32 rows, which show no idle time of their own.

The row of the fine records at the low clock, in the changed kernel:

```profile
49.90 1.93 PE L546 MATMUL ps_four<-t_rows,w_sb 32*32 32x32 f32 x128
```

and the clock beside it:

```profile
50.00:52.00 2.00, 2.00 (x132) 1.94 (x134) 1.86 (x5) 0.11 (x1) 0.00 (x0) 0.50 0.42 73
```

**The sum.** The stops are 7.7 us in both, the matmuls 1.0 less than forecast, the waits 0.2 more, which makes 6.9; between the forecast 79.6 and the measured 86.36 lie 6.8. Rival 4, the slower case, gave the right size (908) for another reason: it wanted 25 us at the low clock, and it was 16.6, whose cost the quicker fine records gave back. Whether the stops lengthen the time at the low clock no run separates; a_bf16, almost without them, still has 12.9 us of it in its loop (a mean of 0.81).

**Behind the boundary** 1 us of gain was forecast. The profiles from group 1 to group 5 show none, and could not: they differ by more than 3 us from one execution to the next.

**What is shown and what is argued.** That the stops are not the matmuls' own is shown by a_late_g2 (same matmuls, no stop after a wait) and by a_shift1 (32 records more, stops 32 records sooner). That each ends with a packet of instructions is shown by the packets' times, 2.2 to 2.9 us ahead of the end in every stop looked up. That fewer records take stops away and save more than the matmuls' own time is shown by a_bf16; it makes the records fewer and the matmuls shorter at once, and a_bf16_rows doesn't continue it. a_cut takes matmuls away as well and can't separate the two. That data hold packets back is shown by a_late_g2 (none for 11 us, the stop 5.76), and borne out by a_late_calm and by two stops of opposite sign in a_busy, in one profile each. That a piece is 128 records long rests on counts (128 records between stops, five more packets for 644 more records, two fewer again in a_bf16 for 256 fewer). The Trainium skill ("Runtime: NRT & Kernel Launch", Instruction fetch mechanics) says that instructions are refilled in 16 KB blocks of 256, fetched over the engine's own DMA queue while it runs. The spacing agrees, since each record has a weight load beside it. It calls the cost of crossing a block "mostly hidden"; here single crossings cost up to 2.86 us in the changed kernel and 5.76 us in a_late_g2, and the measurement decides. Open is what passes between a packet and the first matmul behind it (2.2 to 2.9 us) and why packets come no closer than 3.4 us, why b_shift1 and b_shift2 are 0.3% slower, and what the slow executions of a_nopace are.

## What to carry to other kernels

Count TensorE's instructions as well as its time: a burst of tiny matmuls between two dependencies is paid at the pace at which instructions come, here some 3.5 to 5 us for 128 records, and not at the matmuls' rate. Prefer fewer passes (one-pass types, as in a_bf16; larger tiles should do the same, but were not tried) to faster ones, and keep large loads away from such a burst. A wait ahead of it lets the next piece come in: behind 3.69 us of waiting in a_late_g2 the first stop was gone. When an engine off the path gets a lead, work out first what the engine behind it pays for following; 15 us of VectorE's lead bought nothing here, because TensorE paid 1.5 to 2 us for each 64 small matmuls, and in stops 2 to 3 us more for three of the four bursts.

## What the runs showed of the hardware

- Matmuls of 32x32 on the four diagonal corners in turn overlap: 10.7 ns a record at 2.4 GHz (89 in 0.95 us), 15 ns at 1.2 GHz (128 in 1.93). On the same corner one after the other they take 31.5 ns (89 in 2.80 us, granted clock 1.00) and 50 ns (125 in 6.28 us, granted clock 0.50). The Trainium skill ("TensorE: Matmul & The Clock Gate", Wait — 56ns, not 53.3ns?) states that start-to-start never drops below about 25 ns; for corners in turn the trace has less than half of that.
- TensorE's instruction packets share the DMA engines with data. In ten microseconds at a data share of 0.79 none arrived, and TensorE stood 5.76 us (a_late_g2). A stop ends 2.2 to 2.9 us behind a packet, and on quiet DMA engines packets follow each other in 3.4 to 3.9 us at the closest.
- Stops at the end of a piece lie 128 records apart and fall wherever the count puts them, in the middle of a run of equal matmuls too; the profile calls them "issue". "Issue" can also hide a wait for ScalarE (the 1.68 us ahead of the first u, the 0.74 ahead of the fifth).
